# Attention with expert routing on one core: row and key turning on half arrays, gates summed in PSUM, one scan for all pairs of heads

## The chip, the core and the metric

One Trainium2 chip, one of its cores. The metric is the device time of one execution in microseconds, less is better. The whole computation is one launch of one program.

## The reference

Three stages in fp32: a gated linear attention, a mixture of experts with a greedy capacity routing, and a dense ELU layer.

```python
f = 1.0 / (1.0 + np.exp(-f_logit))                     # q, k, v, f: (4, 8, 768, 48)
for t in range(S):
    state = f[:, :, t, :, None] * state + np.einsum('bhd,bhe->bhde', k[:, :, t], v[:, :, t])
    y[:, :, t] = np.einsum('bhd,bhde->bhe', q[:, :, t], state)
x = y.transpose(0, 2, 1, 3).reshape(B * S, H * D)      # 3072 x 384
logits = x @ w_gate                                    # 8 experts, 384 tokens each
order = np.argsort(-logits.flatten())                  # best first: token to expert, while open and not full
out[mask_e] = np.maximum(x[mask_e] @ w1[e], 0) @ w2[e]
h = out @ w_in                                         # 384 -> 2048
result = np.where(h > 0, h, np.exp(np.minimum(h, 0)) - 1) @ w_out
```

## The kernel before, in words

The change lies in the attention part, the function `attention`. It works on 24 tiles of 128 tokens (4 batches of 6 tiles). In a tile the 8 heads are 4 pairs; the 48 channels of a pair's two heads lie on partitions 0 to 47 and 64 to 111 (HALF is 64, PR is 112), so that a tensor of a tile is 128 x (4 pairs x 128 tokens).

A tile goes through these steps. The letters b and c stand for batch and tile in the batch.

- ScalarE takes exp(-f_logit) (L385, e_x) and adds one (L419, into the PSUM bank growth).
- VectorE scans the running product of growth along the tokens, capped at 1e14, one scan for each pair of heads (L522, rb), and scales the keys with it (L529, k_s).
- ScalarE takes the logarithm of rb (L412), copies its last column for the overflow count (L413, ends), and takes exp(-log) as a guess of the reciprocal (L423). VectorE multiplies rb by the guess (L504, near), GpSimd finishes the Newton step (L318, L324, nb) and scales the queries (L330, q_s).
- TensorE transposes the scaled keys (L623, into kt_ps), ScalarE copies them out (L404, k_tok).
- TensorE makes the scores, 8 products with 48 rows each (L637, a_ps); VectorE masks them (L492, a_m).
- TensorE makes the output from the carried state (L594) and from the tile (L604), both in y_ps, and the tile's part of the new state (L613, ds_ps), which VectorE takes into the state (L481, L483). ScalarE copies y_ps out (L376, x_tr).
- TensorE turns the rows (L580): for each pair one normal fp32 product of x_tr with turn_gate, which holds an identity of 112 columns and behind it the pair's 8 columns of w_gate. So xr_ps gets the tile's rows and, for each pair, a part of the gate logits. ScalarE copies the parts (L367, gate_parts) and the rows (L368, x_row) and issues the store of the rows (L380).

These steps are staggered: in step s of the loop (`run_steps`, 24 steps and a few at the end) the engines work on tile s (exp, growth), s-1 (scan, logarithm), s-2 (Newton, key turning), s-3 (scores, masks), s-4 (output, state) and s-5 (row turning). Each engine goes through its own list of instructions, in an order written out by hand in its function `step`; semaphores are waited for by count. TensorE's order in a step is `turned`, `from_state`, `from_tile`, `state_parts`, `turned_keys`, `scores`. The first tile of a batch has no `from_state`, the last no key turning and no state. The SP queue loads f, k, q and v for the tile six ahead.

The eight PSUM banks are growth, rb, kt_ps, a_ps0, a_ps1, y_ps, ds_ps and xr_ps. Two engines are kept off one bank at a time.

Behind the last step GpSimd adds up gate_parts for the first 20 tiles (L348 to L351), VectorE begins the routing for them (L88 to L94, L100), reduces gate_parts of the last 4 tiles (L565), and goes on with these (L88 again, called from L1704). A product with all_ones counts overflowed tiles (L668); if there were any, a fallback by token, `attention_by_token`, would run. Then come the search for the first expert's tokens (L1277, a product of 8 bf16 columns for each tile, and what is around it) and the expert part, which this change leaves alone but for two waits.

```python
for j in range(pairs):
    ins = nc.tensor.matmul(bank[:, j, 0:PR + experts], x_tr[c % 2][0:PR, j, :], turn_gate[0:PR, j, :], start=True, stop=True)
```

These are the lines of row turning; x_tr is the operand that is loaded as weights, turn_gate the one that is streamed.

Of the kernel before, what the change touches and what calls it, by code (L numbers as in the profile page):

```python
# [23 lines left out]
P = 128  # L24
# [12 lines left out]
def program(nc, q_t, k_t, f_t, v_rows, q_heads, k_heads, f_heads, v_heads, w_gate, gate_rows, w1, w2, w_in, w_out, out):  # L37
# [3 lines left out]
    with ExitStack() as ctx:  # L41
# [20 lines left out]
        def sem(name):  # L62
# [9 lines left out]
        hit_ready = sem("hit_ready")  # L72
        block = ctx.enter_context(nc.Block())
        flag = {}
        attention(nc, block, sem, q_t, k_t, f_t, v_rows, w_gate, w_in, w_out, x_dram, w_in_raw, w_in_hi, w_out_raw, logits, x_row, x_stored,
                  ident, w_in_loaded, w_out_loaded, w_in_upper, overflow, over_known, logits_ready, consts, scan, open_step, hit_ready, flag)
# [3 lines left out]
                       x_row, x_stored, consts, scan, open_step, hit_ready, out)  # L80
# [23 lines left out]
def attention(nc, block, sem, q_t, k_t, f_t, v_rows, w_gate, w_in, w_out, x_dram, w_in_raw, w_in_hi, w_out_raw, logits, x_row, x_stored, ident,  # L104
              w_in_loaded, w_out_loaded, w_in_upper, overflow, over_known, logits_ready, consts, scan, open_step, hit_ready, flag):
# [13 lines left out]
    HALF = 64  # L119
    PR = HALF + dim  # L120
# [3 lines left out]
    with ExitStack() as ctx:  # L124
# [18 lines left out]
        k_tok = [sb(f"k_tok{i}", [P, pairs, P]) for i in range(2)]  # L143
# [3 lines left out]
        gate_parts = sb("gate_parts", [P, tiles, pairs, experts])  # L147
        growth_cap = sb("growth_cap", [P, P])
        turn_gate = sb("turn_gate", [P, pairs, PR + experts])
# [43 lines left out]
        x_ready = sem("x_ready")  # L193
# [9 lines left out]
        logits_begun = sem("logits_begun")  # L203
        gate_read = sem("gate_read")
        flag_turn = sem("flag_turn")
# [19 lines left out]
        def carried(b, c, plus=0):  # L225

            at_c = c + plus
            if at_c < 0:
                return b * CARRY + min(at_c + 1, 0)
            return b * CARRY + min(at_c + 1, CARRY)  # L230

        @block.sync
        def _(sp):
# [31 lines left out]
            for c in range(2, per_batch):  # L265
                load_f(0, c, True)
                load_k(0, c, True)
                load_qv(0, c, True)
                if c == 3:
                    sp.wait_ge(zeros_ready, 2)  # L270
                    for half in range(2):
                        sp.dma_start(turn_gate[half * HALF:half * HALF + dim, :, PR:], w_gate.rearrange("(j u d) e -> u d j e", u=2, d=dim)[half]).then_inc(gate_loaded, 16)
# [15 lines left out]
        def _(pool):  # L288
# [9 lines left out]
            for i in range(2, 6):  # L298
                nc.gpsimd.memset(f_in[i][:], 30.0).then_inc(f_more_pads, 1)
                nc.gpsimd.memset(k_in[i][:], 0.0).then_inc(k_more_pads, 1)  # L300
                nc.gpsimd.memset(q_in[i][:], 0.0).then_inc(q_pads, 1)
                if i == 3:
                    nc.gpsimd.memset(turn_gate[:], 0.0).then_inc(zeros_ready, 1)
                    pool.wait_ge(const_step, 4)
                    pool.wait_ge(zeros_ready, 1)
                    nc.gpsimd.tensor_copy(turn_gate[0:PR, :, 0:PR], ident[0:PR, 0:PR].unsqueeze(1).to_broadcast([PR, pairs, PR])).then_inc(zeros_ready, 1)
# [38 lines left out]
            pool.wait_ge(x_ready, EARLY)  # L345
            pool.sem_inc(nb_turn, 1)
            early = slice(0, EARLY)
            nc.gpsimd.tensor_tensor(gate_parts[:, early, 0, :], gate_parts[:, early, 0, :], gate_parts[:, early, 1, :], ALU.add).then_inc(logits_begun, 1)  # L348
            nc.gpsimd.tensor_tensor(gate_parts[:, early, 2, :], gate_parts[:, early, 2, :], gate_parts[:, early, 3, :], ALU.add).then_inc(logits_begun, 1)
            pool.wait_ge(logits_begun, 2)  # L350
            nc.gpsimd.tensor_tensor(logits[:, early, :], gate_parts[:, early, 0, :], gate_parts[:, early, 2, :], ALU.add).then_inc(logits_begun, 1)  # L351

        @block.scalar
        def _(act):
# [6 lines left out]
            def row_parts(pb, c, bank, reused):  # L361
# [5 lines left out]
                nc.scalar.copy(gate_parts[:, bass.ds(pb * per_batch + c, 1), :, :], bank[:, :, PR:PR + experts].unsqueeze(1)).then_inc(gate_read, 1)  # L367
                nc.scalar.copy(x_row[c % 3][:].rearrange("p (j u d) -> p j u d", u=2, d=dim),  # L368
                               bank[:].rearrange("p j (u d) -> p j u d", u=2)[:, :, :, 0:dim]).then_inc(x_ready, 1)
# [12 lines left out]
            def step(o, b, s):  # L382
# [3 lines left out]
                if 5 <= s:  # L386

                    pb, c = at(b, o, 5)
                    row_parts(pb, c, xr_ps, s >= 6)
# [4 lines left out]
                if 5 <= s:  # L394
                    pb, c = at(b, o, 5)
                    store_rows(pb, c)
                if 2 <= s <= tiles and (o - 2) % per_batch < CARRY:
# [6 lines left out]
                    nc.scalar.copy(k_tok[c % 2][:, :, 0:PR], kt_ps[:, :, 0:PR]).then_inc(ktok_ready, 1)  # L404
                if 1 <= s <= tiles:

                    pb, c = at(b, o, 1)
                    act.wait_ge(k_ready, number(pb, c, 1, 1))

                    if s >= 3:  # L410
                        act.wait_ge(beta_ready, number(pb, c, 1, -1))
                    nc.scalar.activation(guess[c % 2][:], rb[:], ACT.Ln).then_inc(ln_ready, 1)  # L412
                    nc.scalar.copy(ends[:, bass.ds(pb * per_batch + c, 1), :], rb[:, :, P - 1:P].rearrange("p a b -> p b a")).then_inc(end_ready, 1)  # L413
                if s < tiles:
# [4 lines left out]
                    nc.scalar.activation(growth[:], e_x[o % 2][:], ACT.Identity, bias=1.0).then_inc(growth_ready, 1)  # L419
                if 1 <= s <= tiles:  # L420
                    pb, c = at(b, o, 1)
                    act.wait_ge(ln_ready, number(pb, c, 1, 1))
                    nc.scalar.activation(guess[c % 2][:], guess[c % 2][:], ACT.Exp, scale=-1.0).then_inc(guess_ready, 1)  # L423
# [4 lines left out]
            row_parts(end, 3, xr_ps, True)  # L428
            store_rows(end, 3)
            channel_parts(end, 5, True)  # L430
            row_parts(end, 4, growth, True)
            row_parts(end, 5, xr_ps, True)
# [7 lines left out]
        def _(dve):  # L440
# [4 lines left out]
            dve.wait_ge(caps_ready, 1)  # L445
# [25 lines left out]

            def carry_state(pb, c, first):

                s_ap = state[0:PR]
                end = nb[c % 3][0:PR, :, P - 1:P].to_broadcast([PR, pairs, dim])
                dve.wait_ge(ds_done, carried(pb, c))
# [3 lines left out]
                if c > 0:  # L480
                    nc.vector.tensor_tensor(ds_ps[0:PR], ds_ps[0:PR], s_ap, ALU.subtract).then_inc(state_sum, 1)  # L481
                    dve.wait_ge(state_sum, pb * (CARRY - 1) + c)
                nc.vector.tensor_tensor(s_ap, ds_ps[0:PR], end, ALU.mult).then_inc(state_ready, 1)  # L483

            def mask_scores(b, o, s):
                pb, c = at(b, o, 3)
                for par in range(2):
                    dve.wait_ge(a_done, number(pb, c, 2, 2))

                    if s >= 5 and par == 0:  # L490
                        dve.wait_ge(y_made, number(pb, c, 1, -1))
                    nc.vector.tensor_tensor(a_m[c % 2][:, par], a_ps[par][:],  # L492
                                            causal[:].unsqueeze(1).to_broadcast([P, pairs, P]), ALU.mult).then_inc(am_ready, 1)

            def step(o, b, s):
                if 2 <= s <= tiles + 1:

                    pb, c = at(b, o, 2)
                    dve.wait_ge(guess_ready, number(pb, c, 1, 1))
                    dve.wait_ge(end_ready, number(pb, c, 1, 1))  # L500

                    if s >= 4:
                        dve.wait_ge(beta_ready, number(pb, c, 1, -1))
                    nc.vector.tensor_tensor(near[c % 2][:], rb[:], guess[c % 2][:], ALU.mult).then_inc(near_ready, 1)  # L504
                    if s == tiles + 1:
                        dve.wait_ge(near_ready, tiles)
                        dve.wait_ge(beta_ready, tiles - 1)
                        nc.vector.scalar_tensor_tensor(out=nb[c % 3][:], in0=near[c % 2][:], scalar=-2.0, in1=guess[c % 2][:],
                                                       op0=ALU.add, op1=ALU.mult).then_inc(beta_ready, 1)
                        dve.wait_ge(beta_ready, tiles)  # L510
                        dve.wait_ge(y_made, tiles - 3)
                        dve.wait_ge(q_ready, tiles - 1)
                        dve.wait_ge(qv_loaded[c], batches * QV_LOADED)
                        nc.vector.tensor_tensor(q_s[c % 3][:], q_in[c][:], nb[c % 3][:], ALU.mult).then_inc(q_ready, 1)
                if 1 <= s <= tiles:
# [5 lines left out]
                    for j in range(pairs):  # L521
                        ins = nc.vector.tensor_tensor_scan(rb[:, j, :], growth[:, j, :], growth_cap[:], 1.0, ALU.mult, ALU.min)  # L522
                    ins.then_inc(rbeta_ready, 1)
                    dve.wait_ge(rbeta_ready, number(pb, c, 1, 1))
                    dve.wait_ge(k_loaded[c], pb * K_LOADED + K_LOADED)
# [1243 lines left out]
```

## Time and profile before

| | |
|---|---|
| median of 3 runs | 856.23 us (854.91 to 858.41) |
| the profiled execution's own time | 854.62 us |
| its span, first to last instruction | 852.7 us |
| TensorE products busy | 790.8 us, 93% of the span |
| VectorE busy | 493.7 us, 58% |
| ScalarE busy | 465.6 us, 55% |
| GpSimd busy | 528.3 us, 62% |
| mean granted TensorE clock | 0.978 of full speed |

The profile names engines PE (TensorE products), PEld (its loads of weights, which overlap the products), DVE (VectorE), ACT (ScalarE), POOL (GpSimd) and SP (the queue of loads). L580 is line 580 of the kernel before. Times are microseconds, unless ns is said. Ends of products are modelled, their starts are not; an engine's busy time counts overlapping instructions once.

### The profile page before, as it was taken

The page shows a single profiled execution, that of the slowest core. Times are in us where ns is not written, and L with a number is a line of the kernel's source. Part 1 is how long each engine was busy: PE and PEld are TensorE (multiplying, and loading weights), DVE is VectorE, ACT ScalarE, POOL GpSimd, SP SyncE. Part 2 cuts the span into 40 slices and gives each one's busy share as a digit, 9 for nine tenths or more (in the row PEclk, how much of TensorE's full clock was granted, in tenths as well). Part 3 has the DMA queues.
Part 4 walks back from the last instruction along what each step waited for, and adds up shares of the span by engine and source line. Part 5 has one row for each costly group of instructions (what it writes and reads, how often), then busy time and mean ns, then how long its engine had stood idle before and what let it go on. Part 6 is the DMA issues. An engine that isn't in the chain of part 4 may idle for free.

```text
span 852.7 us, 19225 instructions
## 1 busy us (share of the span) xinstructions
PE 790.8 (93%) x6378; PEld 748.9 (88%) x6378; DVE 493.7 (58%) x994; ACT 465.6 (55%) x980; POOL 528.3 (62%) x500
## 2 busy tenths in 40 slices
PE   3999995489999999999999999999999999999995
PEld 2888884378889899989988999899989999999995
DVE  6899998884784476448635764486448426430001
ACT  5677756142664277418732774187428744863653
POOL 8788884477784278527842785278518763964562
PEclk9999997599999999999999999999999999999999
DMA  7777690500410041004100410040004004100000
GB/s 194 208 207 205 195 366 35 184 2 2 148 30 8 23 149 29 13 17 150 28 10 25 148 29 11 19 150 28 20 10 153 25 29 148 28 2 29 1 1 28
DMA packets 33751, 65.83 MB, mean 77 GB/s; under 512 B 4560, under 2 KB 20944, under 8 KB 33280
## 3 DMA queue, kind: packets, MB, share of 16 engines
q1 hardware_dynamic: 27072, 50.36, 18.2%
q0 software_dynamic: 3136, 9.64, 3.5%
q10 hardware_dynamic: 3456, 4.72, 1.6%
q8 instruction: 49, 0.80, 0.4%
q14 instruction: 38, 0.31, 0.1%
HBM read 55.26 MB, written 9.44 MB: 76 GB/s over the span
## 4 chain that ended last, share of the span: by engine, by line
PE 80%; POOL 5%; issue 4%; DVE 4%; ACT 3%; DMA 1%; ACTq 0%; POOLq 0%; SPq 0%; DVEq 0%
PE o_ps L1420 8%; PE o_ps L1421 7%; PE o_ps L1422 7%; PE m_ps L1408 7%; PE m_ps L1409 6%; PE m_ps L1404 6%; PE m_ps L1360 4%; PE o_ps L1378 4%; PE m_ps L1358 4%; PE m_ps L1361 4%; PE o_ps L1380 3%; PE o_ps L1379 3%; PE a_ps L637 3%; PE y_ps L604 3%; PE r_ps L1277 2%
## 5 line engine op out<-in xcount | busy, mean ns | idle before, releaser
L1074 POOL TENSOR_TENSOR t_lo<-whole,t_hi 128x384 fp32r<-128x384 f32 x190 | 203.4, 1072 | 100.1 <-ACT t_hi L1155 98.4
L1102 POOL TENSOR_TENSOR whole<-whole,below 128x384 f32<-128x384 f32 x126 | 133.1, 1057 | 154.2 <-ACT below L1174 153.3
L1408 PE MATMUL m_ps<-y_hi,w_in_hi 128*128 128x384 f32 x384 | 134.4, 350 | 4.3 <-ACT y_hi L1186 4.3
L1420 PE MATMUL o_ps<-w_out_hi,t_hi 128*128 128x384 f32 x378 | 129.7, 343 | 3.4 <-POOL t_lo L1074 2.4
L1409 PE MATMUL m_ps<-y_hi,w_in_low 128*128 128x384 f32 x384 | 129.6, 338 | 0.0
L1421 PE MATMUL o_ps<-w_out_low,t_hi 128*128 128x384 f32 x378 | 127.5, 337 | 0.0
L1422 PE MATMUL o_ps<-w_out_hi,t_lo 128*128 128x384 f32 x378 | 127.1, 336 | 0.0
L1170 ACT ACTIVATE whole<-m_ps 128x384 f32<-128x384 f32 x128 | 62.8, 490 | 93.5 <-PE m_ps L1404 87.3
L1154 ACT ACTIVATE whole<-m_ps 128x384 f32<-128x384 f32 x64 | 31.5, 492 | 130.4 <-PE m_ps L1358 121.0
L1404 PE MATMUL m_ps<-y_lo,w_in_hi 128*128 128x384 f32 x384 | 87.0, 338 | 0.0
L1408 PEld LDWEIGHTS m_ps<-y_hi,w_in_hi 128*128 128x128 f32 x384 | 72.3, 188 | 6.4 <-issue 6.4
L1420 PEld LDWEIGHTS o_ps<-w_out_hi,t_hi 128*128 128x128 f32 x378 | 71.3, 189 | 6.7 <-issue 6.6
L1174 ACT ACTIVATE below<-below 128x384 f32<-128x384 f32 x128 | 67.3, 526 | 16.3
L1409 PEld LDWEIGHTS m_ps<-y_hi,w_in_low 128*128 128x128 f32 x384 | 72.4, 189 | 0.0
L1421 PEld LDWEIGHTS o_ps<-w_out_low,t_hi 128*128 128x128 f32 x378 | 71.2, 188 | 0.0
L1422 PEld LDWEIGHTS o_ps<-w_out_hi,t_lo 128*128 128x128 f32 x378 | 71.2, 188 | 0.0
L1162 ACT CAST t_hi<-whole 128x384 fp32r<-128x384 f32 x128 | 64.0, 500 | 13.1 <-POOL whole L1102 12.0
L1404 PEld LDWEIGHTS m_ps<-y_lo,w_in_hi 128*128 128x128 f32 x384 | 68.9, 189 | 0.0
L1378 PE MATMUL o_ps<-t_hi,w_hi 128*128 128x384 f32 x192 | 67.8, 353 | 1.1 <-POOL t_lo L1074 1.1
L1360 PE MATMUL m_ps<-x_hi,w_hi 128*128 128x384 f32 x192 | 66.4, 346 | 2.1 <-ACT x_hi L1204 1.5
L1380 PE MATMUL o_ps<-t_lo,w_hi 128*128 128x384 f32 x192 | 64.6, 337 | 0.0
L1379 PE MATMUL o_ps<-t_hi,w_low 128*128 128x384 f32 x192 | 64.6, 336 | 0.0
(236 smaller groups left out, 1690.7 us busy)
## 6 DMA issues: line engine op xcount, KB each, us to landing
w_raw<-w SPq DMA_DIRECT2D x16, 1536.0 KB, 7.8
f_in<-f_t SPq DMA_DIRECT2D x48, 96.0 KB, 2.5
k_in<-k_t SPq DMA_DIRECT2D x48, 96.0 KB, 2.6
q_in<-q_t SPq DMA_DIRECT2D x48, 96.0 KB, 2.5
v_in<-v_rows SPq DMA_DIRECT2D x24, 192.0 KB, 2.8
x_scratch<-x_row ACTq DMA_DIRECT2D x24, 192.0 KB, 2.5
w_in_raw<-w_in SPq DMA_DIRECT2D x1, 3072.0 KB, 11.6
w_out_raw<-w_out SPq DMA_DIRECT2D x1, 3072.0 KB, 20.8
```

Source lines behind the costliest of these rows:

```text
L1074: nc.gpsimd.tensor_tensor(t_lo[n % RING][:], whole[n % 3][:], t_hi[n % RING][:], ALU.subtract).then_inc(lo_made, 1)
L1102: nc.gpsimd.tensor_tensor(tile[:], tile[:], below[m % 2][:], ALU.subtract).then_inc(g_made, 1)
L1360: nc.tensor.matmul(m_ps[m % RING][:], w1_hi[:, t, cols], x_hi[:, t, :], start=(t == 0), stop=False)
L1378: nc.tensor.matmul(o_ps[j][:], w2_hi[:, m, cols], hi[:], start=(m == 0), stop=False)
L1379: nc.tensor.matmul(o_ps[j][:], w2_low[:, m, cols], hi[:], start=False, stop=False)
L1380: ins = nc.tensor.matmul(o_ps[j][:], w2_hi[:, m, cols], lo[:], start=False, stop=(m == MH - 1))
L1404: ins = nc.tensor.matmul(bank[:], w_in_hi[:, t, cols], y_lo[:, t, :], start=False, stop=(t == KD - 1))
L1408: nc.tensor.matmul(bank[:], w_in_hi[:, t, cols], y_hi[:, t, :], start=(t == 0), stop=False)
L1409: nc.tensor.matmul(bank[:], w_in_low[:, t, cols], y_hi[:, t, :], start=False, stop=False)
L1420: nc.tensor.matmul(o_ps[t][:], hi[:, rows], w_out_hi[:, m, :], start=(m == 0), stop=False)
L1421: nc.tensor.matmul(o_ps[t][:], hi[:, rows], w_out_low[:, m, :], start=False, stop=False)
L1422: ins = nc.tensor.matmul(o_ps[t][:], lo[:, rows], w_out_hi[:, m, :], start=False, stop=(m == MI - 1))
```

## The change

In place of row turning with the gates in it, TensorE makes the gates by themselves, 4 products of 8 columns that add up in PSUM, and turns the rows by 8 transposes of 48 rows; the keys are turned by 8 such transposes. Rows, gates and keys share two banks (turn_ps), the two halves' scores lie in two banks as before. Row turning waits for the key copy, key turning for the row copy. ScalarE copies 8 finished logits where it copied 32 parts. One scan runs over all four pairs: column 0 of growth holds the cap, and growth_cap holds at column 0 of each pair the growth itself, so that the minimum starts each pair anew; for this the growth copy is split in two. The logarithm waits for the scan instead of the key scaling, which now waits for the end column. ScalarE's order becomes logarithm, ends, key copy, exp, growth. VectorE's becomes scan, state, key scaling, two masks, near, the last for tile s-1 where it was s-2 at the start of the next step. The adds and the reduce of gate_parts go.

```diff
-        k_tok = [sb(f"k_tok{i}", [P, pairs, P]) for i in range(2)]
+        k_tok = [sb(f"k_tok{i}", [P, 2, pairs * dim]) for i in range(2)]
...
-        growth_cap = sb("growth_cap", [P, P])
-        turn_gate = sb("turn_gate", [P, pairs, PR + experts])
+        growth_cap = sb("growth_cap", [P, pairs, P])
+        gate_in = sb("gate_in", [P, pairs, experts])
...
-        kt_ps = ps("kt_ps", [P, pairs, P])
-        a_ps = [ps(f"a_ps{i}", [P, pairs, P]) for i in range(2)]
+        a_ps = ps("a_ps", [P, 2, BANK])
...
-        xr_ps = ps("xr_ps", [P, pairs, P])
+        turn_ps = ps("turn_ps", [P, 2, BANK])
+        HALF_ROW = pairs * dim
+        kt_ps = turn_ps[:, :, 0:HALF_ROW]
+        turned_rows = turn_ps[:, :, HALF_ROW:2 * HALF_ROW]
+        turned_gates = turn_ps[:, 0, 2 * HALF_ROW:2 * HALF_ROW + experts]
...
 GpSimd
-                    nc.gpsimd.tensor_copy(turn_gate[0:PR, :, 0:PR], ident[0:PR, 0:PR].unsqueeze(1).to_broadcast([PR, pairs, PR])).then_inc(zeros_ready, 1)
...
-            nc.gpsimd.tensor_tensor(gate_parts[:, early, 0, :], gate_parts[:, early, 0, :], gate_parts[:, early, 1, :], ALU.add).then_inc(logits_begun, 1)
...
 ScalarE, step
-                if 2 <= s <= tiles and (o - 2) % per_batch < CARRY:
...
-                    nc.scalar.copy(k_tok[c % 2][:, :, 0:PR], kt_ps[:, :, 0:PR]).then_inc(ktok_ready, 1)
                 if 1 <= s <= tiles:
-                    act.wait_ge(k_ready, number(pb, c, 1, 1))
+                    act.wait_ge(rbeta_ready, number(pb, c, 1, 1))
...
                     nc.scalar.activation(guess[c % 2][:], rb[:], ACT.Ln).then_inc(ln_ready, 1)
...
-                    nc.scalar.activation(growth[:], e_x[o % 2][:], ACT.Identity, bias=1.0).then_inc(growth_ready, 1)
+                if 2 <= s <= tiles and (o - 2) % per_batch < CARRY:
...
+                    nc.scalar.copy(k_tok[c % 2][:], kt_ps).then_inc(ktok_ready, 1)
                 if 1 <= s <= tiles:
...
                     nc.scalar.activation(guess[c % 2][:], guess[c % 2][:], ACT.Exp, scale=-1.0).then_inc(guess_ready, 1)
...
+                    nc.scalar.activation(growth[:, :, 1:P], e_x[o % 2][:, :, 1:P], ACT.Identity, bias=1.0)
+                    nc.scalar.activation(growth_cap[:, :, 0:1], e_x[o % 2][:, :, 0:1], ACT.Identity, bias=1.0).then_inc(growth_ready, 1)
...
 VectorE, step
-                    for j in range(pairs):
-                        ins = nc.vector.tensor_tensor_scan(rb[:, j, :], growth[:, j, :], growth_cap[:], 1.0, ALU.mult, ALU.min)
+                    nc.vector.tensor_tensor_scan(rb[:].rearrange("p j t -> p (j t)"), growth[:].rearrange("p j t -> p (j t)"),
+                                                 growth_cap[:].rearrange("p j t -> p (j t)"), 1.0, ALU.mult, ALU.min).then_inc(rbeta_ready, 1)
...
-            then(v.tensor_reduce(logits[:, rest], gate_parts[:, rest].rearrange("p t j e -> p t e j"), AX.X, ALU.add))
...
 TensorE
+            def gates_of(c, gates):
+                for j in range(pairs):
+                    ins = nc.tensor.matmul(gates, x_tr[c % 2][0:PR, j, :], gate_in[0:PR, j, :], start=(j == 0), stop=(j == pairs - 1))
+                return ins
...
+            def rows_of(c, rows):
+                for j in range(pairs):
+                    for par in range(2):
+                        at_head = slice(par * HALF, par * HALF + dim)
+                        ins = nc.tensor.transpose(rows[:, par, j * dim:(j + 1) * dim], x_tr[c % 2][at_head, j, :], ident[at_head, at_head])
...
-                for j in range(pairs):
-                    ins = nc.tensor.matmul(bank[:, j, 0:PR + experts], x_tr[c % 2][0:PR, j, :], turn_gate[0:PR, j, :], start=True, stop=True)
-                ins.then_inc(xr_done, 1)
+                pe.wait_ge(ktok_ready, keys_read)
+                pe.sem_inc(a_turn, 1)
+                gates_of(c, turned_gates)
+                rows_of(c, turned_rows).then_inc(xr_done, 1)
...
+                if rows_read is not None:
+                    pe.wait_ge(x_ready, rows_read)
...
-                    ins = nc.tensor.transpose(kt_ps[:, j, 0:PR], k_s[c % 3][0:PR, j, :], ident[0:PR, 0:PR])
+                    for par in range(2):
+                        rows = slice(par * HALF, par * HALF + dim)
+                        ins = nc.tensor.transpose(kt_ps[:, par, j * dim:(j + 1) * dim], k_s[c % 3][rows, j, :], ident[rows, rows])
...
 routing, VectorE
+                    if fresh and i == 1:
+                        dve.wait_ge(x_ready, tiles)
```

The gate logits of the last two tiles go to columns of rb and growth, their rows to the score banks and turn_ps; the overflow count moves from kt_ps to ds_ps.

## Rows read from the trace of the kernel before

**Rows 1.** The page, busy tenths of TensorE in 40 slices of the span

```profile
PE   3999995489999999999999999999999999999995
```

**Rows 2.** Busy us (instructions) of each engine in one stretch, clock, DMA share, GB/s

```profile
core 0: us, PE busy (x) PEld busy (x) DVE busy (x) ACT busy (x) POOL busy (x), PEclk, DMA share, GB/s
23.00:127.00 104.00, 102.76 (x1528) 90.04 (x1526) 94.24 (x200) 75.31 (x182) 85.70 (x72) 1.00 0.76 235
```

**Rows 3.** The chain of waits, one full step: start us, us, what

```profile
89.99 0.36 PE ds_ps L613 x16
90.34 0.53 PE kt_ps L623 x4
90.88 1.09 PE a_ps L637 x16
91.97 1.08 PE xr_ps L580 x8
93.05 1.01 PE y_ps L594 x16
94.06 1.01 PE y_ps L604 x16
```

**Rows 4.** The chain of waits, a batch's first tile, and the next batch's

```profile
76.16 1.14 PE a_ps L637 x16
...
77.32 0.32 DVE a_m L492
...
78.74 1.08 PE y_ps L604 x16
...
105.23 1.14 PE a_ps L637 x16
```

**Rows 5.** Timelines of PEld in narrow windows: start us, us, instruction, xcount

```profile
131.20 0.19 PEld L668 LDWEIGHTS kt_ps<-over_sum,all_ones 128*128 128x128 f32 x1 [0.18 <-issue]
...
131.31 0.19 PEld L668 LDWEIGHTS kt_ps<-over_sum,all_ones 128*128 128x128 f32 x1
131.51 0.17 PEld L604 LDWEIGHTS y_ps<-a_m,v_in 128*48 128x48 f32 x4
...
90.27 0.20 PEld L623 LDWEIGHTS kt_ps<-ident,k_s 112*128 112x128 f32 x2
...
90.33 0.24 PEld L623 LDWEIGHTS kt_ps<-ident,k_s 112*128 112x128 f32 x2
...
136.09 0.58 PEld L1277 LDWEIGHTS r_ps<-held,slot_hot 128*128 128x128 bf16 x20 [1.70 <-issue]
```

**Rows 6.** Timeline of TensorE's row loads and of ScalarE in the same step

```profile
91.90 0.19 PEld L580 LDWEIGHTS xr_ps<-turn_gate,x_tr 112*128 112x128 f32 x1
...
90.03 0.59 ACT L376 COPY x_tr<-y_ps 112x512 f32<-112x512 f32 x1 [1.09 <-PE y_ps L604]
90.18 0.34 ACTq L380 DMA_DIRECT2D x_scratch<-x_row  x1
90.99 0.53 ACT L404 COPY k_tok<-kt_ps 128x448 f32<-128x448 f32 x1 [0.37 <-PE kt_ps L623]
91.42 0.60 ACT L412 ACTIVATE guess<-rb 128x512 f32<-128x512 f32 x1
91.91 0.17 ACT L413 COPY ends<-rb 128x4 f32 x1
91.95 0.63 ACT L419 ACTIVATE growth<-e_x 128x512 f32<-128x512 f32 x1
```

**Rows 7.** Scans: a group (busy us, mean ns of one | idle before), and a single one

```profile
L522 DVE TENSOR_TENSOR_SCAN rb<-growth,growth_cap 128x128 f32<-128x128 f32 x80 | 27.5, 412 | 2.4 <-DVE near L504 0.5
...
158.49 0.21 DVE L1624 TENSOR_TENSOR_SCAN carry<-r_ps,zero_t 128x24 f32<-128x24 f32 x1
```

**Rows 8.** Timeline of VectorE behind the last mask

```profile
132.38 2.81 DVE L100 TENSOR_TENSOR slot_hot<-best,limit 128x2560 bf16<-128x2560 f32 x1
135.23 0.38 DVE L565 TENSOR_REDUCE logits<-gate_parts 128x32 f32<-128x128 f32 x1
136.07 0.19 DVE L88 TENSOR_REDUCE best<-logits 128x4 f32<-128x32 f32 x1 [0.46 <-DVE logits L565]
```

More of the change, by code:

```diff
@@ L79, in program @@
         route_and_feed(nc, block, sem, w1, w2, x_dram, w_in_raw, w_in_low, w_in_hi, w_in_upper, w_out_raw, w_out_low, logits, ident, w_out_loaded,
-                       x_row, x_stored, consts, scan, open_step, hit_ready, out)
+                       x_row, x_stored, consts, scan, open_step, hit_ready, x_ready, out)
 def begin_tiles(v, then, logits, consts, scan, some, fresh):
@@ L359, in _, with gate_part, row_part @@
                 act.sem_inc(x_stored[i], 1)
-            def row_parts(pb, c, bank, reused):
+            def gate_part(pb, c, gates):
+                nc.scalar.copy(logits[:, bass.ds(pb * per_batch + c, 1), :], gates.unsqueeze(1)).then_inc(gate_read, 1)
+            def row_part(pb, c, rows, reused):
                 act.wait_ge(xr_done, number(pb, c, 1, 1))
@@ L396, in step @@
                     store_rows(pb, c)
+                if 1 <= s <= tiles:
+                    pb, c = at(b, o, 1)
+                    act.wait_ge(rbeta_ready, number(pb, c, 1, 1))
+                    if s >= 3:
+                        act.wait_ge(beta_ready, number(pb, c, 1, -1))
+                    nc.scalar.activation(guess[c % 2][:], rb[:], ACT.Ln).then_inc(ln_ready, 1)
+                    nc.scalar.copy(ends[:, bass.ds(pb * per_batch + c, 1), :], rb[:, :, P - 1:P].rearrange("p a b -> p b a")).then_inc(end_ready, 1)
                 if 2 <= s <= tiles and (o - 2) % per_batch < CARRY:
@@ L427, in _ @@
             channel_parts(end, 4, True)
-            row_parts(end, 3, xr_ps, True)
+            act.wait_ge(xr_done, number(end, 3, 1, 1))
+            gate_part(end, 3, turned_gates)
+            row_part(end, 3, turned_rows, True)
             store_rows(end, 3)
             channel_parts(end, 5, True)
-            row_parts(end, 4, growth, True)
-            row_parts(end, 5, xr_ps, True)
+            for i in range(2):
+                act.wait_ge(gates_done, i + 1)
+                act.sem_inc(row_turn, 1)
+                gate_part(end, 4 + i, spare_gates[i])
+            row_part(end, 4, spare_rows, True)
+            row_part(end, 5, turned_rows, True)
             store_rows(end, 4)
@@ L444, in _ @@
             nc.vector.memset(growth_cap[:], GROWTH_LIMIT).then_inc(caps_ready, 1)
-            dve.wait_ge(caps_ready, 1)
+            nc.vector.memset(growth[:, :, 0:1], GROWTH_LIMIT).then_inc(caps_ready, 1)
+            dve.wait_ge(caps_ready, 2)
             nc.vector.memset(all_ones[:], 1.0)
@@ L480, in carry_state, with mask_scores @@
                 if c > 0:
-                    nc.vector.tensor_tensor(ds_ps[0:PR], ds_ps[0:PR], s_ap, ALU.subtract).then_inc(state_sum, 1)
                     dve.wait_ge(state_sum, pb * (CARRY - 1) + c)
-                nc.vector.tensor_tensor(s_ap, ds_ps[0:PR], end, ALU.mult).then_inc(state_ready, 1)
-            def mask_scores(b, o, s):
+                nc.vector.tensor_tensor(state[0:PR], ds_ps[0:PR], end, ALU.mult).then_inc(state_ready, 1)
+            def mask_scores(b, o, s, par):
                 pb, c = at(b, o, 3)
[L487 to L493, printed above, removed]
@@ L495, in step @@
-            def step(o, b, s):
[L496 to L514, printed above, removed]
@@ new lines, in mask_scores @@
+                dve.wait_ge(a_done, number(pb, c, 2, 1 + par))
+                if s >= 5 and par == 0:
+                    dve.wait_ge(y_made, number(pb, c, 1, -1))
+                nc.vector.tensor_tensor(a_m[c % 2][:, par], a_ps[:, par].rearrange("p (j t) -> p j t", j=pairs),
+                                        causal[:].unsqueeze(1).to_broadcast([P, pairs, P]), ALU.mult).then_inc(am_ready, 1)
+            def step(o, b, s):
+                hands_on = 4 <= s and (o - 4) % per_batch < CARRY
@@ L537, in step @@
                                             accum_out=over_sum[:, 0:1]).then_inc(over_ready, 1)
-                if 3 <= s:
-                    mask_scores(b, o, s)
+                if 1 <= s <= tiles:
+                    pb, c = at(b, o, 1)
+                    dve.wait_ge(rbeta_ready, number(pb, c, 1, 1))
+                    dve.wait_ge(end_ready, number(pb, c, 1, 1))
+                    dve.wait_ge(k_loaded[c], pb * K_LOADED + K_LOADED)
+                    if s >= 4:
+                        dve.wait_ge(a_done, number(pb, c, 2, -4))
+                    nc.vector.tensor_tensor(k_s[c % 3][:], k_in[c][:], rb[:], ALU.mult).then_inc(k_ready, 1)
+                if 3 <= s:
+                    for par in range(2):
+                        mask_scores(b, o, s, par)
+                if 1 <= s <= tiles:
+                    pb, c = at(b, o, 1)
+                    dve.wait_ge(guess_ready, number(pb, c, 1, 1))
+                    if s >= 3:
+                        dve.wait_ge(beta_ready, number(pb, c, 1, -1))
+                    nc.vector.tensor_tensor(near[c % 2][:], rb[:], guess[c % 2][:], ALU.mult).then_inc(near_ready, 1)
             run_steps(dve, step, tiles + 3)
@@ L562, in _ @@
             dve.wait_ge(open_step, count["now"])
-            dve.wait_ge(x_ready, tiles - 1)
             dve.wait_ge(gate_read, tiles)
-            then(v.tensor_reduce(logits[:, rest], gate_parts[:, rest].rearrange("p t j e -> p t e j"), AX.X, ALU.add))
             dve.sem_inc(logits_ready, 1)
@@ L570, in _, with turned @@
             pe.wait_ge(const_step, 4)
-            def turned(pb, c, bank, start, reused):
+            def gates_of(c, gates):
[7 more added lines that the diff above has]
+                        ins = nc.tensor.transpose(rows[:, par, j * dim:(j + 1) * dim], x_tr[c % 2][at_head, j, :], ident[at_head, at_head])
+                return ins
+            def turned(pb, c, start, reused, keys_read):
                 pe.wait_ge(xt_ready, number(pb, c, 1, 1))
@@ L636, in scores @@
                         rows = slice(par * HALF, par * HALF + dim)
-                        ins = nc.tensor.matmul(a_ps[par][:, j, :], k_s[c % 3][rows, j, :], q_s[c % 3][rows, j, :], start=True, stop=True)
+                        ins = nc.tensor.matmul(a_ps[:, par, j * P:(j + 1) * P], k_s[c % 3][rows, j, :], q_s[c % 3][rows, j, :], start=True, stop=True)
                         if j == pairs - 1:
@@ L643, in step @@
                     pb, c = at(b, o, 5)
-                    turned(pb, c, xr_ps, s == 5, number(pb, c) if s >= 6 else None)
+                    kb, kc = at(b, o, 3)
+                    turned(pb, c, s == 5, number(pb, c) if s >= 6 else None, carried(kb, kc))
                 if 4 <= s:
@@ L652, in step @@
                     pb, c = at(b, o, 2)
-                    turned_keys(pb, c, s == 2)
+                    xb, xc = at(b, o, 5)
+                    turned_keys(pb, c, s == 2, number(xb, xc, 1, 1) if s >= 5 else None)
                 if 3 <= s:
@@ L663, in _ @@
             scores(end, 5, False)
-            turned(end, 3, xr_ps, False, number(end, 3))
+            turned(end, 3, False, number(end, 3), batches * CARRY)
             from_state(end, 5, False)
-            pe.wait_ge(ktok_ready, batches * CARRY)
             pe.wait_ge(over_ready, 1)
-            nc.tensor.matmul(kt_ps[:, 0, 0:1], all_ones[:], over_sum[:], start=True, stop=True).then_inc(over_counted, 1)
+            nc.tensor.matmul(ds_ps[:, 0, 0:1], all_ones[:], over_sum[:], start=True, stop=True).then_inc(over_counted, 1)
             from_tile(end, 5, False)
-            pe.wait_ge(rbeta_ready, tiles)
-            turned(end, 4, growth, False, None)
-            turned(end, 5, xr_ps, False, number(end, 4))
+            pe.wait_ge(xt_ready, number(end, 4, 1, 1))
+            pe.wait_ge(near_ready, tiles)
+            pe.sem_inc(a_turn, 1)
+            gates_of(4, spare_gates[0]).then_inc(gates_done, 1)
+            rows_of(4, spare_rows).then_inc(xr_done, 1)
+            pe.wait_ge(xt_ready, number(end, 5, 1, 1))
+            pe.wait_ge(rbeta_ready, tiles)
+            pe.sem_inc(a_turn, 1)
+            gates_of(5, spare_gates[1]).then_inc(gates_done, 1)
+            pe.wait_ge(x_ready, number(end, 4))
+            pe.sem_inc(a_turn, 1)
+            rows_of(5, turned_rows).then_inc(xr_done, 1)
 def attention_by_token(nc, block, sem, q_rows, k_rows, f_rows, v_heads, gate_rows, x_dram, logits, overflow, over_known, logits_ready, x_stored,
@@ L816, in route_and_feed @@
 def route_and_feed(nc, block, sem, w1, w2, x_dram, w_in_raw, w_in_low, w_in_hi, w_in_upper, w_out_raw, w_out_low, logits, ident, w_out_loaded,
-                   x_row, x_stored, consts, scan, open_step, hit_ready, out):
+                   x_row, x_stored, consts, scan, open_step, hit_ready, x_ready, out):
     experts, width, hidden = w1.shape
```

96 lines of the change are left out of this document (50 added, 46 removed).

## The prediction

> **What bounds the kernel now.** I read the page's slices first: TensorE is busy in nine tenths of nearly every slice, and the change touches only the attention part, which ends in the seventh of forty [rows 1]. The stretch from 23 to 127 us, the 21 or so steps in which all stages run, has TensorE busy for 102.76 of 104.00 us at full clock, against 94.24 for VectorE, 85.70 for GpSimd and 75.31 for ScalarE [rows 2]. The chain of waits then shows one full step, and every piece of it is TensorE: state product 0.36, key turning 0.53, scores 1.09, row turning 1.08, product from the state 1.01, product from the tile 1.01, together 5.08 us [rows 3]. So in five of six steps nothing but TensorE's own work counts. The sixth, once a batch, has no product from the state; there TensorE waits for the masks (the chain goes through VectorE between scores and tile product) [rows 4]. From one such step to the same one of the next batch it is 105.23 - 76.16 = 29.07 us, 4.85 us a tile [rows 4]. VectorE is the next bound, and not far away.
>
> **What a product costs.** An fp32 product here is two loads of weights and two streams; a transpose is one of each. Neighbouring loads show what a load of 128 columns takes: the over-count product streams one column, yet its second load starts 0.11 after the first, and the next stage's load, which needs the array drained, 0.20 after the second: 0.11 for the load and 0.09 of draining [rows 5]. For a transpose of 128 columns the second load starts 0.06 after the first (90.27 to 90.33) [rows 5]. Check on row turning: 8 loads at 0.11, the last stream of 120 columns about 0.10, the drain 0.09: 1.07, and the chain says 1.08 [rows 3]. The old row turning is thus as much bound by its 8 loads as by what it streams, and a lighter stream alone wins nothing.
>
> **The change, part by part.**
> *Row turning, gates apart.* Removed: 1.08 a tile. Added: gate products, 4 with x_tr as weights, which are again 8 loads of 128 columns: 8 x 0.11 + 0.09 = 0.97, although each streams 8 columns. Added too: 8 transposes of 48 rows, in pairs on the two halves of the array. Scores run such pairs at 16 loads in 1.09, so two loads go side by side [rows 3]; I take 4 pairs x 0.06, a last stream of 0.04 (48 columns: the 8 pairs of the state product take 0.36, 0.045 each), and 0.09 of draining: 0.37. Together 1.34, 0.26 more than before. It counts for tiles 0 to 20, whose turning stands ahead of the last mask, less 3 in the step where TensorE waits for masks anyway: 18 x 0.26 = **+4.7 us**. Bounds of a gate load: 0.03 (the short bf16 products, 20 loads in 0.58) to 0.13 (turned keys with all their streaming and draining, 0.53 / 4) [rows 3, 5].
> The page "TensorE: Matmul & The Clock Gate" of the Trainium skill, section "Back-to-back issue gap", lets products of 1 to 64 columns follow each other at an issue floor of about 25 ns; by that alone the gates would take 0.20 plus the drain, and this is a rival below. The same page's section "LDWEIGHTS (loading the stationary operand)" counts columns over 1.2 GHz whatever the rows, 107 ns for these, and speaks against the change; the over-count product, with one column, sides with the second.
> *Key turning.* 4 transposes become 8 half ones. Before, with the scores behind it: 0.53 + 1.09 = 1.62. After: 4 pairs x 0.06, the scores' first load 0.11, 8 pairs of streams at 0.112 (0.90), drain 0.09: 1.34; I assume that keys and scores, now on the same halves, need no drain between them. -0.28, for the 17 tiles with keys behind the first three: **-4.8 us**. If a drain stays, -0.19, so -3.2.
> *A new wait.* Keys and rows now share two banks, so row turning waits until ScalarE has copied the keys out, and that copy is moved behind the logarithm and the end column. Counted from the end of the tile product (89.99): TensorE needs state product, keys and scores before the first gate load; before, that load came at 91.90, 1.91 later; now 1.63 [rows 6]. ScalarE starts the x_tr copy at 90.03; its queue then issues the store (90.18 to 90.52) and works off the logarithm's count waits, so the logarithm comes 0.50 to 0.70 after x_tr's start; I take 0.70, since the issue is done only at 0.49. Then 0.49 (91.42 to 91.91) for the logarithm's slot, 0.04 for the ends, 0.53 for the copy: 1.80, with 0.06 to be seen 1.86 [rows 6]. Gates stand 0.23 in front of it, and behind them row products, state and tile products. In 16 steps (keys of tiles 2 to 21 where there are any, less the first): **+3.7 us**; with 0.50 it is 0.5. The other new wait, keys for the row copy, is free: that copy follows turning at once, while two products of 1.01 run.
> *One scan.* 4 scans of 128 take 412 ns each and overlap to 27.5 / 20 = 1.38 a tile. A scan of 24 takes 210, so 104 elements cost 202 ns, and 512 take 412 + 384 x 1.94 = 1157 ns [rows 7]. VectorE gains 0.22 a tile; the path nothing, since TensorE is the bound. Its bounds: 0.9 to 1.4 us.
> *Orders.* VectorE's state before the keys, masks one by one, Newton's product in its own step; ScalarE's logarithm no longer behind the key scaling; the growth copy in two (a small one costs 0.04 to 0.17). All of this has TensorE as cover. Without the cover VectorE sets the step: 104.00 us are 21.4 tiles of 4.85, so it is busy for 94.24 / 21.4 = 4.40 a tile and idle for 0.46 [rows 2]; less 0.22 for the scan and with about 0.4 idle between dependent steps that is 4.6.
> *Set-up and end.* GpSimd's copy into turn_gate and three adds run beside other work: 0. VectorE's last reduce of 0.38 stood between the comparison of 20 tiles, 2.81 long, and the last 4 tiles' search [rows 8]; it goes: **-0.4 us**. The gates of the last tiles come about when that comparison ends, so nothing else is late. SP's queue keeps its transfers and its waits, and the expert part moves as a whole.
>
> **Sum.** 4.7 - 4.8 + 3.7 - 0.4 = +3.2 us. The profiled execution took 854.62 us (span 852.7, 1.9 around it), 1.6 less than the median 856.23 of the runs shown; on the median I expect **859.4 us**, 0.4% more, inside the 0.5% (4.3 us) that a measurement of this kernel can tell from no change. Its own range, by key drain and logarithm's place, is 856 to 862.
>
> **Rivals.**
> *Half transposes don't pair.* For: no transpose before runs on a half array, and only normal products show pairs. Against: the score loads. Place: 8 loads in a row of 0.06 for rows and for keys, +0.24 each; 18 x 0.24 + 17 x 0.24 = +8.4, of which the later keys hide the key-copy wait (3.7): +7.9, **864 us**, slower. It decides as soon as a pair costs over 0.09.
> *Short gates are issue-bound.* For: 20 bf16 products of 8 columns at 0.03. Against: fp32 with one column at 0.11. Then the gates take 8 x 0.03 + 0.09 = 0.33, TensorE falls below VectorE, and VectorE's 4.6 against 4.85 a tile is the step: 20 x 0.25 + 0.4 = 5.4, **851 us**, faster. The skill's issue floor is this case.
> *The key copy is in time.* The logarithm goes right behind x_tr; 3.2 less: **856 us**, no change.
> *Lighter turning is no lighter.* That is my forecast: the change does less than it says, since loads are counted in columns of weights.
>
> **Numbers.** Forecast 0.42 (a quarter of it, 0.10, above 860.5), pairing fails 0.27, gates issue-bound 0.18, copy in time 0.13. Faster by over 0.5%: 0.18; within 0.5%: 0.32 + 0.13 = 0.45; slower: 0.10 + 0.27 = 0.37. The range must reach both outer cases, as either holds more than 1 in 10: 850 to 866, which also takes the worst gate load (18 x 8 x 0.02 = 2.9 above the forecast, 862.3).
>
> **What would show it.** Right: gate loads of 128 columns 0.11 apart, gates near 0.97 and rows near 0.37 in the chain; keys with scores near 1.34; ScalarE's key copy as releaser of 0.2 us before the gates; one scan of 1.16; VectorE idle before the state or key scaling; TensorE busy for nearly all of the steady stretch, which is about 4 us longer. Wrong: gate loads closer than 0.06, or VectorE without gaps (fast case); half transposes one after another, 0.06 or more apart (slow case); the copy done before the scores end.

## The result and the profile after

| | before | after |
|---|---|---|
| median of 12 runs each | 857.23 us | 863.92 us (858.69 to 868.62) |
| profiled execution, its span | 854.62, 852.7 us | 868.62, 866.8 us |
| TensorE busy | 790.8 us | 803.9 us |
| VectorE busy | 493.7 us | 485.6 us |
| mean granted TensorE clock | 0.978 | 0.965 |

The ratio is 1.0077, 95% interval 1.0053 to 1.0101: slower by 0.8%, some 6.6 us. The forecast was 859.4 us, +3.2; the time lies inside the range, but the loss is about twice the forecast one.

The profiled execution is the slowest of the twelve runs of after, 4.7 us over their median; the one before lies 2.6 us under its own. So the spans of the two profiles read below are 14.1 us apart, where the medians are 6.7. Over the twelve runs, the four with a mean granted clock of 0.973 to 0.975 took 858.7 to 859.5 us, the eight with 0.963 to 0.971 took 863.4 to 868.6.

The page of after, busy tenths of TensorE and its granted clock in 40 slices, shows nothing unusual in the attention part (the first seven slices) beside [rows 1]:

```profile
PE   2999999379998999999999999999999999999995
PEclk9999998579999999999999999999999999999998
```

The stretch of [rows 2], first in the kernel after, tells more:

```profile
23.00:127.00 104.00, 100.57 (x1556) 91.22 (x1556) 80.82 (x124) 72.75 (x187) 77.03 (x58) 0.95 0.68 200
```

TensorE, which idled for 1.2 us of the 104 before, now idles for 3.4, and its clock, 1.00 before, is 0.95 in the mean. Three shorter stretches hold the falls, each to the lower of the clock's two levels, 1.2 GHz (it is 0.50 from 55.2 to 58.2, from 86.0 to 88.8 and from 123.5 to 126.3):

```profile
54.00:60.00 6.00, 5.83 (x78) 5.47 (x76) 4.38 (x8) 4.16 (x11) 4.04 (x3) 0.72 0.64 184
85.00:90.00 5.00, 4.95 (x69) 4.65 (x68) 3.73 (x6) 3.55 (x10) 3.91 (x4) 0.66 0.61 168
122.00:128.00 6.00, 6.00 (x81) 5.60 (x79) 3.90 (x8) 3.66 (x10) 4.55 (x4) 0.72 1.00 415
```

The chain of waits in a good step answers to [rows 3]. Keys and scores are 0.38 + 0.96, gates 1.03 (0.99 where they did not wait), rows 0.38:

```profile
77.73 0.38 PE turn_ps L662 x8
78.11 0.96 PE a_ps L676 x16
79.07 0.12 issue
79.19 1.03 PE turn_ps L594 x8
80.22 0.38 PE turn_ps L603 x8
80.60 1.01 PE y_ps L628 x16
81.60 1.03 PE y_ps L638 x16
```

But in the same chain no TensorE stands from 104.14 to 120.65 us, where before it had only a mask or two a batch [rows 4]. The last 14 us of it:

```profile
106.33 1.28 DVE a_m L507 x2
107.61 0.61 DVE near L559
108.31 1.24 DVE rb L518
109.58 0.07 ACT guess L406
...
110.08 0.17 ACT ends L407
110.41 0.07 DVE k_s L548
...
111.62 0.68 DVE a_m L507
112.30 0.61 DVE near L559
...
113.12 1.47 POOL near L323
114.67 1.28 POOL nb L329
...
118.21 1.24 DVE rb L518
...
119.97 0.16 ACT ends L407
120.12 0.39 ACT k_tok L415
120.52 0.14 issue
120.65 1.03 PE turn_ps L594 x8
```

I read it as a ring (e1, e5 and e9 below test the reading): the scan, ScalarE's logarithm and end column, the key scaling behind them, the masks behind that, Newton's product behind the masks, and the next scan. It reaches TensorE at two places, its exits: from the masks to the tile product, and from the end column through the key copy to the gates. The list of waits (total us, times, longest) from 31 to 140 us has a link of the ring, and the second exit:

```profile
DVE k_s L548 <- ACT ends L407: 2.6, 9, 0.4
PE turn_ps L594 <- ACT k_tok L415: 2.5, 7, 0.5
```

*Where the 14.1 us between the two spans are.* The last tile product starts at 143.58, before at 131.51 [rows 5]: 12.1 us lie ahead of it. Clock: 104 x 0.05 = 5.2 us of full speed are lost from 23 to 127. Start: from 23 to 31 us the kernel after issues 80 products, before 116. The profile gives a clock of 1.00 there, but the two output products still take 1.87 and 1.88 us, 1.01 each one step later, so TensorE ran at half its speed until about 31 us:

```profile
25.93 1.87 PE y_ps L628 x16
27.80 1.88 PE y_ps L638 x16
...
33.35 1.01 PE y_ps L628 x16
```

Before, they take 1.01 from 24.73 us on. This costs some 3.5 us (the third tile product comes at 34.3, before at 30.8). The profiled run of e3 below, with the old turning, starts as late (34.3), as do those of e4, e5 and e8 (33.5 to 34.2), and e1 and e2, with the new turning, take 1.01 from 24.9 and 24.6 us on; so this is not the change's doing. The rest, 3.4 us, is work and waits. Behind, 2.0 us: TensorE's last gates, two at half clock, stand ahead of the routing (0.99 each in the steps before):

```profile
145.44 1.88 PE L594 MATMUL rb<-gate_in,x_tr 112*128 112x8 f32 x8
147.25 0.67 PE L603 MATMUL a_ps<-ident,x_tr 48*128 48x48 f32 x8
147.85 1.87 PE L594 MATMUL growth<-gate_in,x_tr 112*128 112x8 f32 x8
```

### The profile page after: what moved, and what is told of

It is laid out like the page before. It is cut to its first block, busy times and chain, and to the rows that moved or that the text cites. A ratio compares the mean times of both kernels' runs of the same rounds, so it can differ in the third digit from the quotient of the medians.

```text
span 866.8 us, 19813 instructions
## 1 busy us (share of the span) xinstructions
PE 803.9 (93%) x6650; PEld 764.6 (88%) x6650; DVE 485.6 (56%) x922; ACT 469.2 (54%) x1004; POOL 527.5 (61%) x496
## 4 chain that ended last, share of the span: by engine, by line
PE 77%; POOL 6%; issue 6%; DVE 4%; ACT 4%; DMA 1%; ACTq 0%; SPq 0%; DVEq 0%; POOLq 0%
PE o_ps L1469 7%; PE o_ps L1471 7%; PE o_ps L1470 7%; PE m_ps L1457 6%; PE m_ps L1458 6%; PE m_ps L1453 6%; PE m_ps L1409 4%; PE o_ps L1427 4%; PE m_ps L1407 3%; PE m_ps L1410 3%; PE o_ps L1429 3%; PE o_ps L1428 3%; PE y_ps L638 3%; PE r_ps L1326 2%; POOL t_lo L1123 2%
```

## The experiments

Ratios are to the kernel before, run on the same chips in the same sessions, with 95% intervals. Its median there was 855.08 us for e1 to e4, 854.55 for e5 to e8 and 854.33 for e9 to e11.

**e1: key copy first.**

```diff
 ScalarE, step
+                    nc.scalar.copy(k_tok[c % 2][:], kt_ps).then_inc(ktok_ready, 1)
...
                     nc.scalar.activation(guess[c % 2][:], rb[:], ACT.Ln).then_inc(ln_ready, 1)
...
-                    nc.scalar.copy(k_tok[c % 2][:], kt_ps).then_inc(ktok_ready, 1)
```

> The kernel after, with ScalarE's key copy back ahead of the logarithm. Theory A (the wait of the gate products for the key copy costs most of the loss): no such wait is left, and the time falls from 864 to about 859, with it the lost clock, since TensorE no longer stands still before the gates. Theory B (the clock drops because turning now streams little, whatever the waits): the wait goes, worth 14 x 0.25 = 3 us at most, but the granted clock in the stretch from 23 to 127 us stays at 0.95 and the time at about 861. Theory C (the gates' loads alone, more work per tile): under 1 us changes, 863.

867.26 us, 1.0133 (1.0100 to 1.0166): slower still, which none of the three theories had. TensorE's wait for the key copy is gone from the list of waits; instead VectorE's key scaling waits for the end column, and TensorE for the masks:

```profile
DVE k_s L548 <- ACT ends L415: 16.1, 19, 1.4
...
PE y_ps L638 <- DVE a_m L507: 3.3, 3, 1.1
```

The chain of e1 shows the path, key copy, logarithm, ends, key scaling, masks:

```profile
115.95 0.04 ACT k_tok L406
...
116.33 0.60 ACT guess L414
116.93 0.06 ACT ends L415
...
117.08 0.07 DVE k_s L548
...
117.68 1.29 DVE a_m L507 x2
```

So the wait was moved, not removed, and the clock stays low, 0.962 to 0.966 in the six runs.

**e2: wide gates.** The gate products stream 104 columns, 8 of w_gate and 96 zeros; the waits stay.

```diff
+        WIDE = 104
-        gate_in = sb("gate_in", [P, pairs, experts])
+        gate_in = sb("gate_in", [P, pairs, WIDE])
...
-        turned_gates = turn_ps[:, 0, 2 * HALF_ROW:2 * HALF_ROW + experts]
+        turned_gates = turn_ps[:, 0, 2 * HALF_ROW:2 * HALF_ROW + WIDE]
```

> The kernel after, with the gate products streaming 104 columns in place of 8, the further 96 being zeros. The loads of weights stay as they are, so the group should stay at 1.03 to 1.1 us. Theory B (little streaming lets the clock fall): the granted clock stays full through the attention part, and the time falls to about 859 to 860. Theory A and Theory C: nothing or up to 1.5 us more, 864 to 865, because only the last stream of each group gets longer. If the zeros count as no activity, B predicts no change either; the trace's clock then stays at 0.95.

861.24 us, 1.0070 (1.0045 to 1.0096), the clock 0.975 to 0.977 in all 7 runs, where after had 0.963 to 0.975. The clock is cured, from 23 to 127 us it is 1.00; the ratio is not told apart from after's.

**e3: orders only**, the kernel before with one scan and the new orders of ScalarE and VectorE. **e4: turning only**, the kernel after with the old orders and four scans. Against the kernel after, e4 goes back so, among other lines (e3 keeps the lines that are taken out here):

```diff
 ScalarE, step
+                    nc.scalar.copy(k_tok[c % 2][:], kt_ps).then_inc(ktok_ready, 1)
...
-                    act.wait_ge(rbeta_ready, number(pb, c, 1, 1))
+                    act.wait_ge(k_ready, number(pb, c, 1, 1))
...
-                    nc.scalar.copy(k_tok[c % 2][:], kt_ps).then_inc(ktok_ready, 1)
...
 VectorE, step
-                    nc.vector.tensor_tensor_scan(rb[:].rearrange("p j t -> p (j t)"), growth[:].rearrange("p j t -> p (j t)"),
+                    for j in range(pairs):
+                        ins = nc.vector.tensor_tensor_scan(rb[:, j, :], growth[:, j, :], growth_cap[:], 1.0, ALU.mult, ALU.min)
...
-                    dve.wait_ge(end_ready, number(pb, c, 1, 1))
```

> The kernel before, with the one scan and the new orders on ScalarE and VectorE, but with the old turning of rows, gates and keys in banks of their own. All theories: TensorE's work per tile is that of before, 5.08 us; no wait for the key copy exists for turning, so within 0.5% of before, 855 to 859. If it is slower by 3 us or more, the orders themselves (the key scaling behind the end column, masks behind it) are part of the loss, against my sum, which put them at nothing.

> The kernel after, with the old orders on ScalarE and VectorE and four scans, so that only TensorE's turning and the shared banks are new. The key copy comes straight behind x_tr there. Theory A: no wait before the gates, so near before, 857 to 859. Theory B: the clock still falls in places, 860 to 863. Theory C, by my sum without the wait: 4.7 - 4.8 - 0.4 = -0.5, so 856 to 857.

e3: 855.87 us, 1.0014 (0.9986 to 1.0042). e4: 853.54 us, 0.9978 (0.9955 to 1.0000). Neither half is told apart from no change: the loss is in their meeting.

**e5: key copy first and masks first**, e1 with one more move:

```diff
 VectorE, step
+                        mask_scores(b, o, s, par)
...
                     nc.vector.tensor_tensor(k_s[c % 3][:], k_in[c][:], rb[:], ALU.mult).then_inc(k_ready, 1)
...
-                        mask_scores(b, o, s, par)
```

> The kernel after with two edits: ScalarE copies the keys out ahead of the logarithm (as in e1_keys_first), and VectorE masks the scores ahead of the key scaling. Theory R (ring): in the new orders either the gates wait for a key copy that stands behind the logarithm, or, with the key copy first, the end column comes late, the key scaling waits for it, and the masks stand behind the key scaling on VectorE. With both edits neither wait reaches TensorE: TensorE busy for over 29.6 of the 30 us from 90 to 120, a full step of about 5.1 us, and a time of 853 to 857 us, ratio near 1.000. Rival N (Newton's product): what makes the new orders slow with the light turning is the late near and GpSimd behind it; nothing of that changes here, so TensorE keeps its waits and the time stays above 861 us.

855.41 us, 1.0003 (0.9981 to 1.0024), within the 853 to 857 expected of theory R, and TensorE has no gap left:

```profile
23.00:127.00 104.00, 103.86 (x1701) 94.39 (x1703) 87.85 (x137) 75.33 (x199) 82.67 (x69) 1.00 0.72 224
```

VectorE's two masks now wait for scores (10.3 us in 20 times), which costs nothing.

**e9: masks first alone**, the diff of e5 on the kernel after, without that of e1: the last corner of the square.

> The kernel after with the masks ahead of the key scaling on VectorE and nothing else; ScalarE's key copy stays behind the logarithm. With e1_keys_first (key copy first alone, 867.26 us) and e5_masks_first (both, 855.41 us) it makes the square of the two moves full. Theory R (both places must be mended): the gates still wait for the key copy, TensorE keeps about 1 us of waits in 30, and the time is 860 to 866 us, ratio 1.006 or more. Rival V (the masks' place was the whole loss, and the key copy's wait costs nothing once the masks are early): 853 to 857 us.

862.83 us, 1.0077 (1.0046 to 1.0107); TensorE waits for the key copy 9 times, 3.3 us. The square of ratios: neither move 1.0077, key copy 1.0133, masks 1.0077, both 1.0003. Each exit of the ring must be shut. In all four near stays where the change put it, so rival N falls with e5.

**e6: copy late**, e4 with ScalarE's key copy moved behind logarithm and ends, nothing else.

```diff
 ScalarE, step
-                    nc.scalar.copy(k_tok[c % 2][:], kt_ps).then_inc(ktok_ready, 1)
...
                     nc.scalar.copy(ends[:, bass.ds(pb * per_batch + c, 1), :], rb[:, :, P - 1:P].rearrange("p a b -> p b a")).then_inc(end_ready, 1)
+                    nc.scalar.copy(k_tok[c % 2][:], kt_ps).then_inc(ktok_ready, 1)
```

> e4_turning_only (light turning, old orders, 853.54 us) with one move: ScalarE's key copy goes behind the logarithm and the end column, VectorE's order stays the old one. Theory R: TensorE's gates wait for the key copy by 0.2 to 0.5 us in about 16 steps, so 857 to 861 us, and waits of TensorE for the key copy show in the list of waits; as the gates are light the clock may fall at times, each fall of about 3.4 us at half clock costing some 1.7 us. Rival V: VectorE's new order is at fault and this move costs nothing: 852 to 855 us.

869.44 us, 1.0181 (1.0162 to 1.0200): one exit of the ring is enough, and dearer than expected, 16 us over e4. The old order has the logarithm behind the key scaling, so near, four scans, key scaling, logarithm, ends and copy all stand ahead of the gates; and the clock falls, to 0.961 to 0.966 in the five runs.

**e10: copy late, wide gates**, e6 with the diff of e2.

> e6_copy_late (869.4 us, seven stretches at half clock before the search) with the gate products streaming 104 columns, 96 of them zeros. The waits stay. Theory C (TensorE's clock falls where waits come on top of short streams): the half-clock stretches go, the granted clock is 0.972 or more against 0.961 to 0.966, and the time falls by 5 to 9 us to 860 to 864 us although the streams cost some 2 us more. Rival (waits alone bring the clock down): the clock stays under 0.968 and the time is 870 us or more.

861.64 us, 1.0070 (1.0045 to 1.0095), 7.8 us under e6. From 60 to 120 us, e6:

```profile
60.00:120.00 60.00, 56.69 (x860) 51.38 (x860) 46.76 (x101) 37.99 (x90) 41.58 (x31) 0.89 0.58 170
```

and e10, where TensorE is busy for no longer and waits as much for the key copy (6.3 us from 31 to 140 us, 6.5 in e6):

```profile
60.00:120.00 60.00, 56.66 (x950) 50.46 (x946) 50.81 (x110) 42.36 (x101) 45.76 (x34) 1.00 0.63 186
```

**e11: e5 with wide gates**, the diff of e2 again.

> e5_masks_first (855.41 us, TensorE without waits) with the wide gate streams: their price where nothing else changes. From e2_wide_gates, whose gates take 1.07 us in the chain where those of e5 take 0.99, 21 x 0.08 = 1.7 us: 856 to 859 us. If gates were bound by what they stream and not by loads, 96 columns more in 8 streams would cost far more than that.

854.82 us, 0.9995 (0.9974 to 1.0015), so a little under what was expected and not told apart from e5. In the chain the gates take 1.07 where e5 has 0.99: 96 more columns in 8 streams cost 0.08 us. The gates are bound by their loads. The pair e2 and e11 sets the kernel after against e5 a second time, both with wide gates and with a clock of 0.975 to 0.977 in all runs: 1.0070 against 0.9995, 0.75%. So the places of key copy and masks cost about as much (0.4 to 1.1% by the two intervals) where no clock is lost.

**e7: orders and the wait**, e3 in which row turning waits for the key copy:

```diff
+                pe.wait_ge(ktok_ready, keys_read)
+                pe.sem_inc(a_turn, 1)
                 for j in range(pairs):
```

> e3_orders_only (old turning in its own bank, new orders, 855.87 us) with one wait more: row turning waits for the key copy, as in the kernel after. Keys and scores take 1.62 us here and not 1.34, so by the numbers of the prediction TensorE comes to row turning 0.05 us behind the key copy: theory R expects a wait under 0.1 us a step and 854 to 858 us, with a granted clock of 0.975 or more. If the wait alone costs what the kernel after lost, it is 859 us or more. If waits alone, and not light streams, bring the clock down, the granted clock falls under 0.970 in some runs.

858.09 us, 1.0042 (1.0023 to 1.0060), just over the 854 to 858 expected. TensorE waits for the copy 3 times, 0.9 us in all, and the clock is 0.972 to 0.979: with the longer keys and scores and the longer row streams the wait alone is small. Whether all of its 0.3% over e3 is that wait stays open; the two intervals overlap.

**e8: e4 with one scan**, the scan lines of e4's diff undone, and the growth copy in two.

> e4_turning_only with the one scan in place of four (and the growth copy in two parts). Theory: VectorE is no bound, so 0.15 us less on it a tile gives nothing: 852 to 856 us, as e4. Rival: the scan is what the new parts need, and it gives 20 x 0.15 = 3 us: 850.5 us.

856.26 us, 1.0003 (0.9983 to 1.0022). No gain of the scan is to be seen in the time; the group in the kernel after is

```profile
L518 DVE TENSOR_TENSOR_SCAN rb<-growth,growth_cap 128x512 f32<-128x512 f32 x19 | 23.4, 1231 | 1.8
```

No version clearly beats the kernel before; e4 comes nearest, with an interval that ends at 1.0000.

## Why the prediction was half right

- **Row turning, gates apart (+0.26 a tile): right.** 0.99 and 0.38 against 0.97 and 0.37, so +0.29. e11 shows the gates bound by loads, so the rival of issue-bound gates falls; 8 half transposes in 0.38, where 0.37 + 0.24 = 0.61 was forecast if they do not pair, show pairs, so that rival falls too.
- **Key turning (-0.28): right**, keys and scores take 0.38 + 0.96 = 1.34 us to the hundredth, so no drain between them.
- **These two and the end together, -0.5 us:** e5 and e8, with light turning and one scan and no waits, measure +0.3 us (1.0003), within their intervals of 2 us: in line with it, though so small a gain could not be told from none.
- **One scan: right in effect** (0), a little low in size, 1.23 against 1.16 us.
- **The new wait (+3.7) and the orders (0): the step that failed.** The wait is there, as forecast, though not evenly: 2.5 us in 7 steps, 0.36 us at a time, where the sum had 0.23 in each of 16. But "all of this has TensorE as cover" costed the orders at nothing. That held in e3, whose TensorE has the old turning, and not together with the shared banks. After less e5 is 1.0077 - 1.0003, that is 0.74% or 6.3 us, for the places of key copy and masks alone, where the sum had 3.7. By the two intervals it can be 3.6 to 9.1 us, so the size alone does not refute the sum; e1 does: the rival "the key copy is in time" had 856 us for it, and with the key copy ahead of the logarithm the kernel took 867.26. The prediction added VectorE's work (4.6 against 4.85 a tile) and never followed the handshake scan, logarithm, end column, key scaling, masks, which ties VectorE to ScalarE in the same step; in e1 VectorE waits for its end column for 16.1 us, where the kernel after has 2.6.
- **The clock, taken as unchanged: failed too, its size in the median open.** In the profiled run it is up to 5.2 us from 23 to 127 us. The runs show what it takes for a fall: in e4, e5 and e8 the short streams are there and TensorE does not wait (busy for 103.7 to 103.9 of 104 us), in e2 and e10 it waits and the gate streams are long, and the clock from 23 to 127 us is 1.00 in all five; with waits and short streams it is 0.95 in the kernel after, 0.97 in e9, 0.90 in e1 and 0.89 in e6. How the 6.6 us of the medians divide stays open, as two readings differ: by e2 and e11 the waits cost all of it at full clock, while in the twelve runs of after the time goes with the clock, some 6 us between the four with the highest and the other eight, and no trace of those four says whether they waited less too. The Trainium skill, page "TensorE: Matmul & The Clock Gate", Part 4 (PE-mode transpose), states that transposes do not count as TensorE being busy in the way that products do. No run here shows it: none has the transposes alone, and e5, with all of them, keeps 1.00.
- **End (-0.4): wrong sign in the profiled run.** 2.0 us more, since the last gates ran at half clock.

## What to carry over

An engine that was busy 99% did not cover this edit, because the waits among the others closed into a ring that reached it at two places; when an operation is made to wait within a step, list what stands behind it on its own engine, for both places to which it can be moved. Two edits that each measure as no change can cost 0.8% together, so after each alone, test the meeting. Where a tight TensorE schedule gets shorter streams, look at the granted clock before the busy time.

## What was not expected of the hardware

- TensorE, busy for 94% in both e6 and e10, 56.69 and 56.66 of 60 us, was granted 0.89 of its clock with gate streams of 8 columns and 1.00 with 104, mostly zeros. In this pair streaming zeros is faster: 869.44 against 861.64 us.
- 96 more columns in each of 4 fp32 products cost 0.08 us for the four, under loads of 128 columns of weights.
- Transposes of 48 rows on the two halves of the array run in pairs: in the kernel after their loads start two at a time, at 91.08, 91.14, 91.20 and 91.26 us, and 8 take 0.38 us, where 4 of 112 rows took 0.53.
